# Expert 1's first weight quarter moved into attention, and two gathers moved behind expert 2's first cast loads

## What is computed

```python
# attention: q, k, v of shape (4, 8, 576, 64)
scores = q @ k.T / sqrt(64)
scores = where(scores >= max(scores) - tau, scores, -1e9)
attn = softmax(scores); x = attn @ v              # as 2304 tokens x 512
# mixture of experts: 8 experts, top 1, D 512, F 1024
logits = (x / |x|) @ (emb / |emb|).T / moe_tau
e = argmax(logits); gate = softmax(logits)[e]
x = gate * (relu(x @ w1[e]) @ w2[e])
# dense layer, F2 = 2048
h = x @ w_in
out = (h * tanh(softplus(h))) @ w_out
```

## Time and profile before

| | us |
|---|---|
| median of 3 runs | 1097.88 (1097.64 to 1098.24) |
| the profiled execution, its own time | 1094.31 |
| the span that its profile covers | 1092.6 |
| TensorE busy | 1033.4 (95%) |
| VectorE busy | 629.5 (58%) |
| ScalarE busy | 504.7 (46%) |
| GpSimd busy | 583.7 (53%) |

### The profile page before, as it was taken

One profiled execution on the slowest core, in us unless ns is written; L12 is line 12 of the kernel. 1 busy time (PEld: TensorE's weight loads), 2 busy tenths in 40 slices (PEclk: granted clock), 3 DMA queues, 4 the chain that ended last, 5 costly groups with the idle time before them and its releaser, 6 DMA issues.

```text
span 1092.6 us, 20910 instructions
## 1 busy us (share of the span) xinstructions
PE 1033.4 (95%) x6712; PEld 858.3 (79%) x6712; DVE 629.5 (58%) x1455; ACT 504.7 (46%) x1019; POOL 583.7 (53%) x672
## 2 busy tenths in 40 slices
PE   7999999999949999799999985899999999999998
PEld 5777777777627887688888874799998999989997
DVE  6888888988653221121222124567767667676664
ACT  5777777777552222122222212354554545545553
POOL 3344344433348776776630606876556565565554
PEclk9999999999968999899999997999999999999999
DMA  8145432441267889888834507401001010010000
GB/s 210 45 114 166 118 98 61 118 128 52 78 208 226 284 245 305 284 274 292 279 120 184 173 20 212 116 11 58 1 1 59 1 58 0 0 58 0 30 1 29
DMA packets 97525, 128.84 MB, mean 118 GB/s; under 512 B 34400, under 2 KB 51808, under 8 KB 96928
## 3 DMA queue, kind: packets, MB, share of 16 engines
q1 hardware_dynamic: 72976, 67.32, 20.9%
q0 software_dynamic: 18880, 53.22, 15.6%
q10 hardware_dynamic: 5584, 7.16, 1.9%
HBM read 111.69 MB, written 15.99 MB: 117 GB/s over the span
## 4 chain that ended last, share of the span: by engine, by line
PE 59%; DMA 5%; POOL 5%; issue 2%; DVE 2%; ACT 1%; POOLq 0%; SPq 0%; ACTq 0%; DVEq 0%
PE ps L1048 18%; PE ps L1050 18%; PE ps L1049 18%; DMA stage<-w 4%; POOL wl L560 3%; PE ps L1074 1%; PE ps L1123 1%; PE ps L988 1%; PE ps L1044 1%; POOL wh L571 1%; DVE mn L1449 1%; PE ps L998 1%; POOL xs_far L597 0%; ACT junk L778 0%; DMA yg<-y_sorted,gidx 0%
## 5 line engine op out<-in xcount | busy, mean ns | idle before, releaser
L560 POOL TENSOR_TENSOR wl<-stage,wh 128x512 fp32r<-128x512 f32 x128 | 161.9, 1290 | 56.7 <-DMA stage<-w 52.3
L672 POOL TENSOR_TENSOR mg<-mw,mr 128x384 f32<-128x384 f32 x96 | 118.5, 1234 | 75.1 <-DVE mr L1468 75.0
L720 ACT ACTIVATE ex<-sc,rmin 128x576 f32<-128x576 f32 x144 | 111.6, 776 | 78.3 <-DVE sc L1244 78.3
L1048 PE MATMUL ps<-yth,winh 128*128 128x384 f32 x384 | 133.0, 346 | 8.8 <-DVE mw L1456 8.8
L676 POOL TENSOR_TENSOR gl<-mg,gh 128x384 fp32r<-128x384 f32 x96 | 97.6, 1016 | 78.3 <-ACT gh L847 78.3
L1050 PE MATMUL ps<-yth,winl 128*128 128x384 f32 x384 | 130.9, 341 | 0.0
L1049 PE MATMUL ps<-ytl,winh 128*128 128x384 f32 x384 | 130.6, 340 | 0.0
L1254 DVE SCALAR_TENSOR_TENSOR pm<-sc,thr,ex 128x576 f32<-128x576 f32 x144 | 116.2, 811 | 20.0 <-POOL thr L526 15.1
L1244 DVE TENSOR_SCALAR_CACHE_REDUCE sc<-ps,nscale 128x576 f32<-128x576 f32 x144 | 116.8, 813 | 10.2 <-PE ps L897 9.6
L526 POOL TENSOR_SCALAR thr<-rmin,taup 128x1 f32<-128x1 f32 x144 | 71.4, 497 | 85.0 <-DVE sc L1244 83.7
L1050 PE MATMUL ps<-wouth,gl 128*128 128x512 f32 x288 | 114.0, 396 | 0.0
(11 more groups left out here) (187 smaller groups left out, 2304.7 us busy)
## 6 DMA issues: line engine op xcount, KB each, us to landing
stage<-w SPq DMA_DIRECT2D x128, 256.0 KB, 4.6
wh<-w POOLq DMA_DIRECT2D x32, 1024.0 KB, 8.5
y_sorted<-yo ACTq DMA_DIRECT2D x25, 256.0 KB, 4.2
q_t<-qT SPq DMA_DIRECT2D x16, 288.0 KB, 3.6
k_t<-kT SPq DMA_DIRECT2D x16, 288.0 KB, 3.8
vb<-v SPq DMA_DIRECT2D x16, 288.0 KB, 4.5
out<-os SPq DMA_DIRECT2D x18, 256.0 KB, 4.2
stage<-w_in SPq DMA_DIRECT2D x16, 256.0 KB, 3.2
```

The lines of the kernel that those rows point to most:

```text
L560: g.tensor_tensor(dst, raw, src.bitcast(F32), ALU.subtract).then_inc(w_split, 1)
L672: g.tensor_tensor(mg[:, f % 2, :], mw[:, f % 2, :], mr[:, f % 2, :], ALU.mult).then_inc(g_done, 1)
L720: act.activation(ex[:, i % 2, t * S:(t + 1) * S], sc[:, i % 2, t * S:(t + 1) * S], ACT.Exp, bias=rmin[:, i % 2, t:t + 1], scale=-1.0).then ...
L1048: pe.matmul(out_, lhs_h, rhs_h, start=start, stop=False)
```

## The change

Four things are changed. The timetable inside attention is denser and longer: a split every 3 units and no longer every 4, for 20 chunks and no longer 16, so that the last four are expert 1's quarter 0; its cast load is issued behind unit 43; SP issues its chunks one body earlier. To make room for these weights, the attention buffers are placed elsewhere (`q_t` in two tensors, `k_t` behind the constants, `xtr` in other halves). At the end of attention GpSimd issues three cast loads instead of four, and splits quarters 1 and 2 of expert 1 instead of 0 and 1. The gathers of slots 18 and 19 go behind the first two cast loads of expert 2, in the place where quarter 2 of expert 1 was split, with a semaphore `x_next` of their own.

```diff
@@ -55,6 +55,7 @@
 NEAR = 15
 IN_X = 10
 AHEAD = NT + 2
+FAR = NT
 ROUND = 1.5 * 2 ** 23
 
 E, F = 8, 1024
@@ -145,20 +146,26 @@
     stage = sb("stage", [P, STAGES, CHUNK], F32, end)
     AFTER = end[0]
 
-    mid = [WB + HALF]
-    q_t = sb("q_t", [P, BUFS, S], F32, mid)
-    k_t = sb("k_t", [P, BUFS, S], F32, mid)
+    q_t = [None] * 2
+    mid = [WB + HALF + HALF // 4]
     sc = sb("sc", [P, 2, W2], F32, mid)
     ex = sb("ex", [P, 2, W2], F32, mid)
+    q_t[0] = sb("q_t0", [P, HEADS, S], F32, mid)
+    assert mid[0] <= WB + 2 * HALF
+    mid = [WB + 2 * HALF + HALF // 4]
     pm = sb("pm", [P, 2, W2], F32, mid)
     pt = sb("pt", [P, 2, W2], F32, mid)
+    q_t[1] = sb("q_t1", [P, HEADS, S], F32, mid)
     ot = sb("ot", [P, 2, P], F32, mid)
     assert mid[0] <= WB + 3 * HALF
 
-    sta = [WB + 2 * HALF + HALF // 2]
+    WIDE = [n for n in range(XRING) if n % RG < RG - 1]
+    sta = [WB + 3 * HALF - HALF // 4]
     xtr = [None] * XRING
-    for n in range(0, XRING, 2):
-        xtr[n] = sb(f"xtr{n}", [P, (RT if n % RG < RG - 1 else NT % RT) * P], F32, sta)
+    for n in WIDE[0::2]:
+        xtr[n] = sb(f"xtr{n}", [P, RT * P], F32, sta)
+    assert sta[0] <= WB + 3 * HALF
+    sta = [WB + 3 * HALF - HALF // 4]
     lgt = sb("lgt", [P, RT * P], F32, sta)
     lgt_l = sb("lgt_l", [P, (NT % RT) * P], F32, sta)
     lmax2 = sb("lmax2", [P, NT], F32, sta)
@@ -204,11 +211,14 @@
     lane_b = sb("lane_b", [P, P], BF16, sta)
     lane_f = sb("lane_f", [P, P], F32, sta)
     kept = sta[0]
+    k_t = sb("k_t", [P, BUFS, S], F32, sta)
+    sta = [kept]
     z = sb("z", [P, NT, E], F32, sta)
     incl = sb("incl", [P, E, NT], F32, sta)
     pref = sb("pref", [P, E, NT], F32, sta)
-    for n in range(1, XRING, 2):
-        xtr[n] = sb(f"xtr{n}", [P, (RT if n % RG < RG - 1 else NT % RT) * P], F32, sta)
+    for n in range(XRING):
+        if n not in WIDE[0::2]:
+            xtr[n] = sb(f"xtr{n}", [P, (RT if n in WIDE else NT % RT) * P], F32, sta)
 
     xr = [X0]
     xth = sb("xth", [P, KD, P], F32R, xr)
@@ -312,6 +322,7 @@
     x_first = [sem(f"x_first{i}") for i in range(FIRST)]
     x_near = sem("x_near")
     x_far = sem("x_far")
+    x_next = sem("x_next")
     x_last = sem("x_last")
     gates_kept = sem("gates_kept")
     xg_in = sem("xg_in")
@@ -407,10 +418,13 @@
         return BODY * (H // HEADS + k + 1)
 
     def low_after(c):
-        return BODY + 4 * c
+        return BODY + 3 * c
 
     def high_after(j):
         return 3 + 10 * j
+
+    EARLY = CH_E + CQ
+    assert low_after(EARLY) < NUNIT
 
     def route_tiles(gr):
 
@@ -429,7 +443,7 @@
     def _(sp):
         def load(t):
             buf = t % BUFS
-            sp.dma_start(q_t[:, buf, :], q_rows[t]).then_inc(qk_in[buf], 16)
+            sp.dma_start(q_t[buf // HEADS][:, buf % HEADS, :], q_rows[t]).then_inc(qk_in[buf], 16)
             sp.dma_start(k_t[:, buf, :], k_rows[t]).then_inc(qk_in[buf], 16)
             sp.dma_start(vb[:, buf, 0:TPP, :], v_rows[t].rearrange("(c p) d -> p c d", p=P)).then_inc(v_in[buf], 16)
             even = t % HEADS == 0
@@ -471,12 +485,13 @@
             t0 = (b - 1) // (H // HEADS)
             sp.dma_start(x_rows[:, t0 * TPP:(t0 + 1) * TPP, c0 * P:(c0 + 1) * P],
                          x[:, t0 * TPP:(t0 + 1) * TPP, c0 * P:(c0 + 1) * P]).then_inc(x_stored, 16)
-            while issued < CH_E and low_after(issued - STAGES) < b * BODY:
-                expert_chunk(0, issued)
+            while issued < EARLY + CQ and low_after(issued - STAGES) < (b + 1) * BODY:
+                expert_chunk(issued // CH_E, issued % CH_E)
                 issued += 1
 
-
-        with sp.Fori(1, E) as e:
+        for c in range(issued, 2 * CH_E):
+            expert_chunk(1, c - CH_E)
+        with sp.Fori(2, E) as e:
             expert(e)
         win_c = w_in.rearrange("(k p) (c f) -> c p k f", p=P, c=CH_E)
         wout_c = w_out.rearrange("(c p) n -> c p n", p=P)
@@ -539,9 +554,11 @@
                 for j in range(QUARTERS):
                     if unit(b, i) == high_after(j):
                         load_quarter(0, 0, j)
-                for c in range(CH_E):
+                if unit(b, i) == high_after(QUARTERS):
+                    load_quarter(1, 1, 0)
+                for c in range(EARLY):
                     if unit(b, i) == low_after(c):
-                        low_chunk(0, 0, 1, c)
+                        low_chunk(c // CH_E, c // CH_E, 1, c % CH_E)
 
         w1_e = w1.rearrange("e (k p) f -> e p k f", p=P)
         w2_e = w2.rearrange("e (c p) n -> e p c n", p=P)
@@ -587,13 +604,13 @@
         for b in range(NITER):
             attention(b)
         g.wait_ge(normed, NUNIT)
-        for i in range(QUARTERS):
+        for i in range(1, QUARTERS):
             load_quarter(1, 1, i)
-        for i in range(2):
+        for i in range(1, 3):
             low_quarter(1, 1, 1, i)
 
         def gather(s):
-            got = x_first[s] if s < FIRST else x_near if s < NEAR else x_far if s < AHEAD else x_last
+            got = x_first[s] if s < FIRST else x_near if s < NEAR else x_far if s < FAR else x_next if s < AHEAD else x_last
             g.indirect_dma_start(x_slot(s), None, x_tok, bass.IndirectOffsetOnAxis(inv_i[:, s:s + 1], 0),
                                  bounds_check=N - 1, oob_is_err=False).then_inc(got, 16)
 
@@ -603,7 +620,7 @@
         for s in range(NEAR):
             gather(s)
         g.wait_ge(gates_kept, 1)
-        for s in range(NEAR, AHEAD):
+        for s in range(NEAR, FAR):
             gather(s)
         g.wait_ge(routed, 1)
 
@@ -615,7 +632,8 @@
             load_quarter(e, par, 0)
             load_quarter(e, par, 1)
             if isinstance(e, int) and e == 2:
-                low_quarter(e - 1, 1 - par, n - 1 + par, 2)
+                for s in range(FAR, AHEAD):
+                    gather(s)
             low_quarter(e - 1, 1 - par, n - 1 + par, 3)
             low_quarter(e, par, n, 0)
             g.wait_ge(m2_done, first)
@@ -885,7 +903,7 @@
                             rows = slice(lane * DH, lane * DH + DH)
                             to = (lane + t) % LANES * DH
                             q0 = (1 - lane) * PAIRS * P
-                            m = pe.matmul(s_psum(t)[to:to + DH, h, :], q_t[rows, st + t, q0:q0 + DH],
+                            m = pe.matmul(s_psum(t)[to:to + DH, h, :], q_t[st // HEADS][rows, t, q0:q0 + DH],
                                           k_t[rows, st + t, h * S // 2:(h + 1) * S // 2], start=True, stop=True)
                         if h == 1:
                             m.then_inc(scores_done, 1)
@@ -894,7 +912,7 @@
                 for lane in range(LANES):
                     rows = slice(lane * DH, lane * DH + DH)
                     q0 = r % PAIRS * P + lane * DH
-                    m = pe.matmul(s_psum(lane)[:, h, :], q_t[rows, st, q0:q0 + P],
+                    m = pe.matmul(s_psum(lane)[:, h, :], q_t[st // HEADS][rows, st % HEADS, q0:q0 + P],
                                   k_t[rows, st, h * S // 2:(h + 1) * S // 2], start=True, stop=True)
                     if h == 1:
                         m.then_inc(scores_done, 1)
@@ -1034,7 +1052,9 @@
             elif i == FIRST:
                 pe.wait_ge(x_near, 16 * (NEAR - FIRST))
             elif i == NEAR:
-                pe.wait_ge(x_far, 16 * (AHEAD - NEAR))
+                pe.wait_ge(x_far, 16 * (FAR - NEAR))
+            elif i == FAR:
+                pe.wait_ge(x_next, 16 * (AHEAD - FAR))
             elif i == AHEAD:
                 pe.wait_ge(x_last, 16 * (SLOTS - AHEAD))
             rows = x_slot(i)
```

## The result

The changed kernel takes 1087.19 us (median of 4 runs, 1084.41 to 1088.63), the kernel before 1097.76 (4 runs, 1097.04 to 1098.24) beside it. The ratio is 0.9901, 95% interval 0.9881 to 0.9922: 10.6 us faster, where I had forecast 6.6. The time lies just inside the lower end of the range.

A forecast was written before the change was run, and what follows sets the result against it. Bound: GpSimd's splits and SP's reloaded chunks in turn, making TensorE wait at slots 7 and 9. Expert stage 6.2 + attention 0.4 = 6.6 us won, from the median 1097.88 to 1091.3 us; range 1087.0 to 1096.0.

The forecast's parts named there:

- The bound, its two places: Expert stage: TensorE waits for GpSimd's splits at slots 7 and 9, 2.17 and 6.19 us, losing 13.39 us together.
- the head start: GpSimd at expert 2: fewer splits and two gathers behind the first cast loads bring the second cast loads 5.5 us earlier.
- the 0.4: Attention: 0.4 us won, between -0.4 and 0.8, as unit 13 loses its paired cast load and split.
- the row and the rule: Attention: by trace rows a split costs its unit 0.14 us, given back; by SBUF exclusion four more could cost 5.2.
- the wait for `m2` of slot 1: Expert 2's second cast loads: this wait, ending at 363.40 us, takes over, so nothing earlier can be won.
- slot 7's wait: TensorE's wait for expert 3's quarter 1 split: gone with 3.5 us to spare, 4.05 us won.
- From there on: GpSimd's rounds after expert 2's second cast loads: rows unchanged, so the 5.5 us gain carries on to experts 3 and 4.
- S: How much earlier expert 2's second cast loads start: 5.5 us, at best 6.5, at worst 3.2.
- both waits vanish: Rival, expert stage: TensorE's waits at slots 7 and 9 both go, 13.39 + 0.4 us won, 1084.1; chance 0.08.
- the median of the runs is 1097.88, and with the same difference: Final sum: profiled 1094.31 becomes 1087.7 us; the same 6.6 us off the 1097.88 median gives 1091.3.
- The rival by DMA: Rival, 349 to 448 us: bytes count, not splits, so DMA gives part back; 4.1 us won, 1093.8; chance 0.18.
- The two slower ones: Rivals: splits hold attention's masking, 1101.7, chance 0.06; gathers stall behind cast loads, 1101.0, chance 0.04.

The follow-up runs named there:

- quarter_only: The changed kernel with gathers 18 and 19 back ahead of expert 2's first cast loads; ratio to the kernel before 0.9942.
- a_third: The changed kernel, unaltered, for a third profile; its profiled execution took 1079.39 us.
- a_again: The changed kernel, unaltered, run again beside the kernel before; ratio 0.9904, profiled execution 1083.72 us.
- the clean pair: Third profiles of the kernel before and the changed kernel, unaltered, in one set, neither with the stop; 1094.15 and 1079.39 us.
- late_second: The changed kernel with the last split of expert 2's quarter 0 done four times, same result; ratio to the kernel before 0.9976.
- half_chunks: The kernel before with SP loading only the first half of each raw chunk of experts 1 to 7; ratio 0.9932.
- b_again: The kernel before, unaltered, for one more profile; its profiled execution took 1095.76 us.
- timetable_only: The kernel before with only attention's timetable changed: sixteen splits, one every 3 units, SP's chunks a body earlier; ratio 0.9988.
- gathers_late: The changed kernel with the gathers of slots 20 to 24 issued behind expert 5, not expert 2; ratio to the kernel before 0.9874.
- pause_gathers: The changed kernel with gathers of slots 20 to 24 behind expert 5 and of slots 10 to 14 behind the `gates_kept` wait; ratio to before 0.9900.

## Why the prediction was wrong in its size

**Held.** The bound, its two places, and the way in which the head start comes about. In attention the cast loads at its end start at 293.54, 293.56 and 293.49 us in three profiles of the changed kernel, and at 293.91, 293.98 and 293.71 before, 0.3 us earlier on average. That fits the 0.4 and doesn't prove it, for with the same attention quarter_only has 293.92. Units with a split give it back (3.94 + 3.67 = 7.61 us), so of the row and the rule that were weighed against each other the row was right. By the rule of the Trainium skill (page "SBUF — State Buffer", section "SBUF: two separate sides") four more splits could have cost 5.2 us, an estimate; attention did not end later. Gathers behind cast loads were issued in 1.06 and 1.05 us, the wait for `m2` of slot 1 took over where it was expected in two profiles of three (0.67 us in a_third, 1.96 in a_again), and slot 7's wait was gone. The first product of slot 0 came at 328.81 us (329.56 in a_third, 329.19 before).

**The step that failed** is *From there on*: "the rows are the same as before, so I carry S along". From the second cast loads on, before took 77.3 to 79.8 us in three profiles and the changed kernel 73.1 to 75.4 in three. So S did not stay 5.5. In the clean pair it was 10.6 us against the rows of the prediction (447.92 to 437.33), the wait at slot 9 was 0 where I said 4.7, and the stage lost 0.0 us where I said 7.2. This is my rival *both waits vanish*, at 0.08. I had put it low because "a later round would have to win nearly 4 us by itself". The later rounds together won 4.9. The rows that I had could have told that a round isn't a fixed length: two like places already gave 9.1 and 9.6 us to a first chunk, and DMA was at 0.89. late_second shows that the effect goes both ways: 3.9 us taken away bring back the long stretch (77.3) and cost 8.1 us, where carried on they would have cost 5 to 6. The times alone hardly tell these apart (5.8 to 10.4), so the weight lies on the stretch.

**A second step**, *the median of the runs is 1097.88, and with the same difference*: the profiled execution of before was 3.6 us faster than its median (1094.31 and 1097.88) and has no stop; that of the changed kernel has the stop, and is at its median (1087.24 and 1087.19). My 1087.7 for the profiled execution looks right, and that is luck: 3.6 us lost in slots 0 and 1 hide that slots 2 to 9 won 9.5 and not 6.2. That before's slower executions have the stop is likely and not shown, since only profiled executions can be looked into.

The rival by DMA was right in that bytes count (half_chunks), and wrong in sign: the later loads landed sooner, not later. The two slower ones did not appear.

**Open.** Why the loads land sooner when GpSimd comes early to expert 3. The profiles split by that start, late_second moves one kernel across by time alone, and no run shows what in the queues differs. The place of the stores is not shown, and whether the change's two parts only work together isn't either.

## What to carry to other kernels

Where GpSimd's own work and the loads behind it take turns, don't shift the rows of before by a constant: give the later rounds a range (here 73 to 80 us for the same bytes), and let the forecast's range end where all waits are gone, with more than a small chance. Price a head start against the wait that it removes. Look at the intervals before you call two edits more than their sum: here one at a time they measured 0.7 and 6.4 us, together 10.5, and the runs leave open whether the 3.4 us between are real. And compare the profiled execution with the runs' median before summing against it. If they differ by 3.6 us, what it lacks may be just what the changed kernel's profile has.

## What the runs showed of the hardware

ScalarE and VectorE stopped at slot 0 for some 2 to 6 us, behind a releaser that the trace calls "remote". Here is VectorE in b_again, and below it what DMA moved in 40 slices of 336 to 347 us:

```profile
339.64 0.69 DVE L1405 TENSOR_TENSOR xtl<-ps,xth 128x512 fp32r<-128x512 f32 x1 [6.43 <-issue]
344.82 0.18 DVE L1396 COPY gsum<-ps 128x25 f32<-128x25 f32 x1 [4.48 <-remote]
...
GB/s 149 89 179 372 164 104 179 194 328 149 149 119 223 283 179 104 194 283 194 179 238 209 313 149 179 149 223 283 149 179 119 313 283 75 15 60 0 0 0 0
```

DMA is busy with the gathers during the whole stop, and falls from 283 GB/s to nothing between 345.1 and 345.9 us, just after VectorE goes on at 344.82. In six more profiles with the stop (the changed kernel's, a_again, quarter_only, timetable_only, late_second, gathers_late) VectorE also goes on 0.4 to 0.9 us before the last of the gathers' bytes have moved. That fits the theory of pause_gathers, that the stop lasts until the queue of gathers has drained, and doesn't prove it.

12 of the 18 experiments and the changed kernel's first profile have the stop, 6 and before's first don't. It goes by sets: in each of the five sets all kernels have it or none, whatever their code. It lengthens slots 0 and 1 by 1 to 4 us and puts GpSimd's first cast loads of expert 2 some 2.4 to 3.6 us later (349.13 and 349.22 against 346.73 in the changed kernel, 352.42 against 348.82 and 349.07 before). What the engines wait for was not shown.
